# Delta-rule attention and two dense layers: own bank for state changes, fewer zero-state products, VectorE work in other slots, first keys on two queues

## The reference

```python
k_n = k / (norm(k) + 1e-06)
for t in range(S):
    y[:, :, t] = q[:, :, t] @ state
    v_old = state applied to k_n[:, :, t]
    state = state + beta * outer(k_n[:, :, t], v - v_old)
x = y as (3072 tokens, 384)
h = x @ w_in;  g = 0 for h <= -1, h for h >= 1, (h + 1)^2 / 4 between;  x = g @ w_out
h = x @ w_in2; g = max(h, 0)^2;  result = g @ w_out2
```

## Time and profile before

| | us |
|---|---|
| median of 3 runs | 1066.27 (1064.67 to 1068.62) |
| profiled execution, its time | 1071.0 |
| its span, first to last instruction | 1069.1 |
| PE busy | 995.6 (93%) |
| DVE busy | 608.9 (57%) |
| before `residual(0)` | 44.04 |
| slots 0 to 6 (first `residual` to `residual(7)`) | 89.5 |
| mean granted TensorE clock | 0.953 of full |

### The profile page before, as it was taken

One profiled execution on the slowest core, in us unless ns is written; L12 is line 12 of the kernel. 1 busy time (PEld: TensorE's weight loads), 2 busy tenths in 40 slices (PEclk: granted clock), 3 DMA queues, 4 the chain that ended last, 5 costly groups with the idle time before them and its releaser, 6 DMA issues.

```text
span 1069.1 us, 24504 instructions
## 1 busy us (share of the span) xinstructions
PE 995.6 (93%) x10528; PEld 822.9 (77%) x10528; DVE 608.9 (57%) x1150; ACT 398.2 (37%) x712; POOL 25.4 (2%) x43
## 2 busy tenths in 40 slices
PE   3246799999999999999999999999999999999997
PEld 3245678888888888888888888888888888888886
DVE  5887878887777777644544577343433434334332
ACT  3123334444434333433433455333323333333322
POOL 2100000000000000000000000000000000000000
PEclk7557689999999999999999999999999999999999
DMA  4422333312122111210100251101001010000000
GB/s 133 155 75 87 96 98 98 95 42 86 39 67 80 39 49 39 76 38 19 51 2 1 95 172 59 60 1 49 11 1 60 1 59 1 1 30 1 30 1 30
DMA packets 30251, 56.79 MB, mean 53 GB/s; under 512 B 2496, under 2 KB 16320, under 8 KB 30144
## 3 DMA queue, kind: packets, MB, share of 16 engines
q1 hardware_dynamic: 30144, 55.22, 16.5%
HBM read 45.78 MB, written 9.44 MB: 52 GB/s over the span
## 4 chain that ended last, share of the span: by engine, by line
PE 89%; DVE 5%; issue 2%; ACT 1%; ACTq 0%; DVEq 0%
PE psum L868 37%; PE psum L844 37%; PE psum L711 3%; PE psum L753 2%; PE psum L716 2%; PE psum L692 2%; PE psum L739 2%; PE psum L798 1%; DVE tmp L961 1%; PE psum L776 1%; PE psum L781 1%; PE psum L789 1%; PE psum L677 1%; DVE x_inv L964 1%; DVE w L1047 1%
## 5 line engine op out<-in xcount | busy, mean ns | idle before, releaser
L844 PE MATMUL psum<-x_hi,w 128*128 128x512 f32 x1152 | 388.7, 392 | 1.5 <-DVE x_lo L1055 1.5
L868 PE MATMUL psum<-g_hi,w 128*128 128x512 f32 x1152 | 389.6, 393 | 0.0
L1075 DVE TENSOR_TENSOR g_lo<-act_g,g_hi 128x512 fp32r<-128x512 f32 x192 | 132.7, 691 | 233.6 <-ACT g_hi L592 233.6
L844 PEld LDWEIGHTS psum<-x_hi,w 128*128 128x128 f32 x1152 | 217.0, 188 | 49.0 <-issue 1.6
L868 PEld LDWEIGHTS psum<-g_hi,w 128*128 128x128 f32 x1152 | 216.2, 188 | 48.3 <-issue 2.2
L592 ACT ACTIVATE g_hi<-act_g 128x512 fp32r<-128x512 f32 x192 | 121.3, 632 | 301.4 <-PE psum L868 235.4
L844 PE MATMUL psum<-x_lo,w 128*128 128x512 f32 x576 | 225.0, 391 | 0.0
L868 PE MATMUL psum<-g_lo,w 128*128 128x512 f32 x576 | 224.5, 390 | 0.0
L1069 DVE TENSOR_TENSOR act_g<-act_g 128x512 f32<-128x512 f32 x96 | 66.4, 692 | 112.1 <-ACT act_g L585 112.1
L844 PEld LDWEIGHTS psum<-x_lo,w 128*128 128x128 f32 x576 | 108.6, 189 | 22.0
L868 PEld LDWEIGHTS psum<-g_lo,w 128*128 128x128 f32 x576 | 108.2, 188 | 21.3
(11 more groups left out here) (73 smaller groups left out, 618.6 us busy)
## 6 DMA issues: line engine op xcount, KB each, us to landing
kt_sb<-in_k_t SPq DMA_DIRECT2D x24, 256.0 KB, 2.9
qt_sb<-in_q_t SPq DMA_DIRECT2D x24, 256.0 KB, 3.3
ring<-in_v_s SPq DMA_DIRECT2D x27, 192.0 KB, 2.5
kt_ahead<-in_k_t SPq DMA_DIRECT2D x10, 512.0 KB, 4.1
kn_sb<-in_k_n SPq DMA_DIRECT2D x20, 256.0 KB, 4.5
between_layers<-y_out SPq DMA_DIRECT2D x6, 768.0 KB, 3.3
x_sb<-between_layers SPq DMA_DIRECT2D x6, 768.0 KB, 5.6
result<-y_out SPq DMA_DIRECT2D x6, 768.0 KB, 4.2
```

What stands on the lines that cost most here:

```text
L844: ins = pe.matmul(h_ps[n % 2][:, :], w_in_part(layer, f // GW, part)[:, kt, fs], x[:, kt, :], start=(kt == 0 and j == 0), stop=(kt == KT - ...
L868: ins = pe.matmul(acc[kt][:, :], w_out_part(layer, f // GW, part)[:, f % GW, ds], g[n % 2][:, :], start=(f == 0 and j == 0), stop=(f == NF ...
L1075: dve.tensor_tensor(g_lo[n % 2][:, :], act_g[n % 2][:, :], g_hi[n % 2][:, :].bitcast(F32), ALU.subtract).then_inc(g_lo_ready, 1)
```

## The change

Five edits, all in the part up to slot 7.

- The state changes of items 0 to 3 go to bank 4 (`ds_ps(m)`), and `state_change` of those waits for the first copy to `u_sb` of its slot, not for all four.
- `substitute` leaves out the products of keys with the state for chunk 0's blocks 1 to 3, where the state is zero; the first product with `gram` then starts the accumulation. Block 0 of each item is still multiplied.
- The inverse of chunk 2 (`n == 2`, slots 4 to 7) is laid out anew by `late_inverse`: `start_inverse` comes a quarter later, the last quarter of slots 5 and 6 holds none of it, and slot 7 holds pieces 6 to 10 and the transposition in place of pieces 9 and 10 and the transposition.
- Groups 0, 1 and 2 are split in quarter 1 of slots 4, 5 and 6, on both engines; it was in slots 0, 1 and 2. The load of group 2, which reuses a staging tile, moves along.
- Chunk 0's keys are loaded by two transfers of two batches each, one issued by SP and one by ACT, ahead of ACT's first activation.

```diff
-        t_ps = s_ps = ds_ps = bank[6]
+        t_ps = s_ps = bank[6]
+        def ds_ps(m):
+            return bank[4] if m + NB - 1 < SERIAL else bank[6]
...
-            for m in range(B):
-                load_kt(m)
+            sp.dma_start(kt_sb[:, 0:2, :, :], k_t[0][:, 0:2 * HP, :].rearrange("p (b a) t -> p b a t", b=2)).then_inc(kt_first[0], 16)
...
-                if s == 0:
+                if s == B:
                     load_weights(0, 2, w_in1, w_out1)
...
+            act.dma_start(kt_sb[:, 2:B, :, :], k_t[0][:, 2 * HP:B * HP, :].rearrange("p (b a) t -> p b a t", b=2)).then_inc(kt_first[1], 16)
...
-                    if q == 3 and s < EARLY:
-                        split_weights(0, s, 0)
-                        split_weights(0, s, 1)
+                    if q == 1 and B <= s < B + EARLY:
+                        split_weights(0, s - B, 0)
+                        split_weights(0, s - B, 1)
...
-                pe.wait_ge(kt_loaded[b], 16)
+                pe.wait_ge(kt_first[b // 2], 16)
...
                     for m, i in going:
+                        if i and m < B:
+                            continue
                         ins = by_state(m, i, a)
...
-                                            u_of(m % B * H + j), start=False, stop=(j == H - 1))
+                                            u_of(m % B * H + j), start=(j == 0 and m < B), stop=(j == H - 1))
...
-                pe.wait_ge(u_ready, before(m + NB))
+                if m + NB - 1 < SERIAL:
+                    pe.wait_ge(u_ready, before(m + NB - 1) + 1)
+                else:
+                    pe.wait_ge(u_ready, before(m + NB))
...
+                        pe.wait_ge(state_ready, 2 * (SERIAL - NB + 1))
...
-                if at == 2 and not half_of:
+                if at == (3 if n == 2 else 2) and not half_of:
                     start_inverse(n)
+                if n == 2:
+                    late_inverse(n, at, half_of)
+                    return
...
+            def late_inverse(n, at, half_of):
+
+                if at in (4, 5, 6, 8, 9, 10):
+                    pieces(n, at - 4 - at // 8, half_of)
+                if at == 12:
+                    pieces(n, 6, half_of)
+                if at in (13, 14):
+                    inverse_steps(n, PIECES[2 * at - 19 + half_of], PIECES[2 * at - 18 + half_of])
+                if at == 15 and not half_of:
                     turn_inverse(n)
...
-                    if q == 1 and s < EARLY:
-                        split_weights(0, s, 0)
-                        split_weights(0, s, 1)
+                    if q == 1 and B <= s < B + EARLY:
+                        split_weights(0, s - B, 0)
+                        split_weights(0, s - B, 1)
```

More of the change, by code:

```diff
@@ L188, in delta_rule_then_two_moe @@
         beta_loaded = sem("beta_loaded")
+        kt_first = [sem(f"kt_first{i}") for i in range(2)]
         kt_loaded = [sem(f"kt_loaded{i}") for i in range(KEYS)]
@@ L680, in gram_of @@
             def gram_of(m):
-                pe.wait_ge(kt_loaded[m % KEYS], 16 * (m // KEYS) + 16)
+                pe.wait_ge(kt_loaded[m % KEYS], 16 * (m // KEYS) + (16 if m % KEYS >= B else 0))
                 if m <= SERIAL:
@@ L794, in state_change @@
                 pe.wait_ge(kn_loaded[m % 2], 16 * (m // 2 + 1))
-                pe.wait_ge(u_ready, before(m + NB))
+                if m + NB - 1 < SERIAL:
+                    pe.wait_ge(u_ready, before(m + NB - 1) + 1)
+                else:
+                    pe.wait_ge(u_ready, before(m + NB))
                 for a in range(HP):
                     for hp in range(2):
-                        ins = pe.matmul(ds_ps[hp * DP:(hp + 1) * DP, a * D:(a + 1) * D], kn_sb[:, m % 2, 2 * a + hp, :],
+                        ins = pe.matmul(ds_ps(m)[hp * DP:(hp + 1) * DP, a * D:(a + 1) * D], kn_sb[:, m % 2, 2 * a + hp, :],
                                         u_of(m % B * H + 2 * a + hp), start=True, stop=True)
@@ L1002, in new_state @@
                     s = s_bd[part, pairs_of(m % B), hp, :]
-                    dve.tensor_tensor(s, s, ds_ps[part, 0:HP * D].rearrange("p (a e) -> p a e", e=D), ALU.add
+                    dve.tensor_tensor(s, s, ds_ps(m)[part, 0:HP * D].rearrange("p (a e) -> p a e", e=D), ALU.add
                                       ).then_inc(state_ready, 1)
@@ L1037, in ahead @@
                 if at == 14 and not half_of:
+                    turn_inverse(n)
+            def late_inverse(n, at, half_of):
[6 more added lines that the diff above has]
+                if at == 15 and not half_of:
                     turn_inverse(n)
```

## The result

| | before | changed |
|---|---|---|
| median of 6 runs, us | 1068.12 (1064.67 to 1069.38) | 1072.58 (1071.83 to 1074.80) |
| profiled execution, us | 1071.0 | 1072.45 |
| span, us | 1069.1 | 1070.6 |

The ratio of changed to before is 1.0052, 95% interval 1.0034 to 1.0070: the changed kernel is about 5 us slower (4.5 us between the medians). The forecast was +2.7 us (1069.0, range 1061 to 1076).

What follows compares the result with a forecast made beforehand. PE was the busy engine over the whole span, but DVE's queue bound slots 0 to 2 and a DVE-PE relay the later ones. Terms summed to +2.7 us on the 1066.3 us median: 1069.0 us, range 1061 to 1076.

Steps and rivals of the forecast that it cites:

- likeliest case: Whole kernel: gain and loss nearly cancel, within 0.5% of before; 1069 us, range 1063 to 1071.6, chance 0.5.
- second rival: Ends of slots 4 to 6 and slot 7: PE at half clock behind longer pauses, slower, some 1074 us; chance 0.3.
- `clamp(0)` to `solve(8)`: Start of the dense layer: moved inverse steps, +4.3 us, plus PE at half clock behind its pause, +1.7 us.
- Splits out of slots 0 to 2: Slots 0 to 2: 3.71, 1.74 and 1.74 us leave DVE's own path to the residual; -7.2 us, nothing hiding it.
- Slot 4: Slot 4: split replaces `start_inverse`, while a 1.65 us PE stall may not recur; -0.5 us, bounds -1.25 and +1.7.
- +0.4 later: Slot 4: `new_state` is 0.4 us later because a 1.74 us split replaces `start_inverse`, some 1.3 us.
- Slots 5 and 6: Other inverse pieces plus the split delay `new_state` by 2.13 and 1.91 us; terms +1.9 and +1.5 us.
- Slot 7: Ahead of `gram_of(8)`: 6.75 us of steps added, transposition moved behind; +4.3 us, PE's pause growing to about 5 us.
- The clock's term: Behind PE's pause in slot 7: work at half speed for 3.4 us, costing +1.7 us, bounds none to 4.
- Keys on two queues: Kernel start: PE needs the first 512 KB, not 256 KB; +1.0 us, between no loss and +2.0.
- Bank 4 and the zero-state products: `state_change` and `substitute` on PE: DVE makes `new_state` late and block 0's chain stays; cost and gain 0.
- The base: Sum put on the runs' median, 1066.27 us; the profiled execution, 1071.0 us, lay 4.7 above it.

Runs made afterwards that it cites:

- VectorE part alone: Kernel before with only the splits of groups 0 to 2 moved to slots 4 to 6 and chunk 2's inverse laid out anew: 1072.25 us, ratio 1.0038.
- second profile: Profile from a second series of the kernel before, unchanged: series median 1067.51 us, ratio 1.0000; profiled span 1065.7 us.

## Why the prediction came out right, and where it was off

The direction, the range and the mechanism held. The number is partly luck. By its ratio the rise is 0.52% (0.34 to 0.70) where the likeliest case said "within 0.5%", and 1072.58 lies above that case's 1071.6: it falls where the second rival, with its chance of 0.3, had it. Half of the way from 1069.0 to 1072.58 is the median of before, 1066.27 us in three runs and 1068.12 in six. What that rival names, work at half speed behind the pauses, is there in part: in slot 7 it cost 1.6 us in the changed kernel's profile and 2.8 in that of the VectorE part alone. And the terms have errors of both signs: slot 7 too large, slot 4 and the TensorE edits too small. Term by term, against the first profile of before (the one that the prediction used) and against the second:

| term | forecast | first profile | second profile |
|---|---|---|---|
| start to `residual(0)` | +1.0 | +0.7 | +1.4 |
| slots 0 to 2 | -7.2 | -7.3 | -7.3 |
| slot 3 | 0 | -0.2 | -0.2 |
| slot 4 | -0.5 | +1.1 | +2.8 |
| slot 5 | +1.9 | +0.8 | +2.4 |
| slot 6 | +1.5 | +0.6 | +1.0 |
| `clamp(0)` to `solve(8)` | +6.0 | +4.5 | +4.5 |
| sum | +2.7 | +0.3 | +4.6 |

The spans differ by 1.5 and 4.9 us; what the sums lack, 1.2 and 0.3 us, lies behind `solve(8)`, where nothing was changed.

- *Splits out of slots 0 to 2.* Right to 0.1 us: DVE's queue alone decided there.
- *Slot 4.* This term was mis-sized. The forecast counted on a stall of PE going away. The second profile of before has none, so there was nothing to win against a usual run. The "+0.4 later" was right where PE is no later: in the VectorE part alone `new_state` came 8.48 us behind the residual against 7.96, and slot 4 took 11.60 us, 0.7 more than the second profile's 10.87; in the changed kernel without steps 17 to 24 it took 11.66. The 13.69 us of the changed kernel's profile, with `new_state` at 10.02, are an execution in which DVE waited 1.78 us for PE ahead of the mask, at a mean clock of 0.66. So some 0.7 of the +2.8 in the table is DVE's work; the rest goes with the clock of that execution.
- *Slots 5 and 6.* The later `new_state` was right in sign; it came 10.38 and 10.36 us behind the residual, not 12. The sum counted DVE's work alone and left out that DVE had waited for PE ahead of the mask, 1.61 and 1.69 us in the first profile, and that more work ahead eats that wait; in the changed kernel 0 and 0.45 us of it were left. Against the second profile, where slot 5 had no such wait, slot 5's step is 10.38 - 8.25 = 2.13 us, the forecast's own number. What is lost against a usual run is +2.4 and +1.0, near the terms. In the VectorE part alone `new_state` came 10.91 and 11.90 us behind. Slots 4 to 6 together take 41.4 to 41.9 us in the three kernels with this layout and these splits, 2 us more than in the first profile of before and 6 more than in the second, where the three terms say +2.9.
- *Slot 7.* The mechanism was right and the size of one term too large. Counted from `clamp(0)`, `gram_of(8)` starts 17.84 us behind it and not 14.93, so 2.9 us later where the forecast had 4.3. The forecast let `gram_of(8)` hang on `new_state`, behind all the moved steps. But PE's pause is ended by ACT's copy, and this hangs on `activated(2)`, which moved by the same 2.91 us (15.75 against 12.84 behind `clamp(0)`). Steps 28 to 30 stand behind `activated(2)`, 151.18 to 152.62: these 1.44 us were counted, but do not stand ahead of what ends the pause. The clock's term, 1.7 us, was right: from `gram_of(8)` to `solve(8)` it is 10.25 us against 8.68, 1.6 more. The VectorE part alone has the same 17.84 and then 11.50, so its slot 7 is 5.7 us longer; how long the low clock lasts differs from one profile to the other. That 1.7 fits is luck in part, since it was taken from 3.4 us in which PE had no work at all. Leaving out the moved steps takes the pause away and 6.2 us with it.
- *Keys on two queues.* The first matmul came at 5.67, within 4.04 to 6.0 and near its upper end. The edit alone costs 0.21% (0.04 to 0.37), and the three profiles with it have `residual(0)` 1.5 us later in the mean, between the middle and the upper end. The Trainium skill ("DMA: Bandwidth & Descriptors", Issuing engines are not separate DMA queues) says that transfers issued by several engines run on the same 16 DMA engines and that only the time of issuing is saved. The trace agrees: both were issued at 0.80 us, by two engines, and PE still waited to 5.67 us.
- *Bank 4 and the zero-state products, forecast at nothing.* Together they cost 0.22% (0.09 to 0.35). This term was missed. That they gain nothing was right: `substitute` begins its `gram` products sooner, and DVE was late anyway. Why they cost is open. Both go along with more executions at a low mean clock (above), and the means are 0.950 for both edits and 0.956 for the unchanged kernel. But the edit of bank and wait leaves PE all its work, and raising the clock with extra products brought no time, so the clock as the cause is only argued.
- *The base.* The sum was a difference to one profiled execution, and put on the median without asking where that execution's extra 4.7 us lay. Against the second profile, 3.4 us shorter, slots 4 to 6 hold all of the difference, the very slots in which three terms were sized.

## What to carry to other kernels

Work moved off one stage's critical engine has to land in a wait of that engine, not in a later stage that looks less busy: three splits of 1.74 us each, with the wait of 1.96 us that the first brought, won 7.3 us by leaving slots 0 to 2. They were largely paid again ahead of the one instruction that slots 4 to 6 hang on (1065.66 us), and cost nothing that shows in waits of the same length (1060.95 us). When a wait is priced, find the instruction that ends it: only the work ahead of that one counts. Before a stage's share is read from one profile, read a second of the same kernel: a relay between two engines can differ by 3.7 us in 39 with the program unchanged. Here the first matmul waited 1.6 us longer for the first of two 512 KB transfers than for the first of four of 256 KB; that size and not the second queue is the reason was not tried apart.

## What was not expected of the hardware

- With extra matmuls in the pauses the granted TensorE clock of slots 3 to 6 went from 0.74 to 0.90 and the kernel was no faster (1060.99 against 1060.95 us, in two series; ratios 0.9934 and 0.9918).
- PE stalled 1.65 us in the middle of `substitute` in one execution of the kernel before and not in another of the same program (slot 4: 12.57 and 10.87 us). Nothing in the trace names a cause.
- Two edits that only take waits and products away from PE made the kernel 0.22% slower (0.09 to 0.35), with a mean clock below 0.950 in 4 of 9 executions and in 1 of 89 of the unchanged kernel.
